# A mixer kernel in which the turns of the spatial gating weights are placed anew on TensorE

## The reference

```python
def _moe2_ref(x, w_in, g_ln, w_sg, b_sg, w_out) -> np.ndarray:
    h = x @ w_in
    c = np.float32(np.sqrt(2.0 / np.pi))
    h = 0.5 * h * (1.0 + np.tanh(c * (h + 0.044715 * h ** 3)))
    d_ff = h.shape[-1]
    u, v = (h[..., :d_ff // 2], h[..., d_ff // 2:])
    mu = np.mean(v, axis=-1, keepdims=True)
    var = np.mean((v - mu) ** 2, axis=-1, keepdims=True)
    v_n = (v - mu) / np.sqrt(var + 1e-06) * g_ln
    v_s = np.einsum('ts,bsd->btd', w_sg, v_n) + b_sg[None, :, None]
    gated = u * v_s
    return (x + gated @ w_out).astype(np.float32)
```

## Time and profile before

| | |
|---|---|
| time, median of 3 runs (lowest to highest) | 716.33 us (715.87 to 718.21) |
| the profiled execution's own time | 717.76 us |
| its span, first to last instruction | 715.9 us |
| PE busy | 706.1 us (99%) |
| DVE, ACT, POOL busy | 483.6, 382.8, 357.9 us |
| mean granted clock of TensorE | 0.998 of full speed |
| chain that ended last | PE 90%, DVE 7% |

### The profile page before, as it was taken

How to read it: one execution, slowest core, us unless ns; L and a number is a source line. 1 busy time by engine, 2 the same in 40 slices (tenths; PEclk the granted TensorE clock), 3 DMA queues, 4 the chain that set the end, 5 groups by cost and what they waited for, 6 DMA issues and landing times.

```text
span 715.9 us, 11889 instructions
## 1 busy us (share of the span) xinstructions
PE 706.1 (99%) x3933; PEld 596.4 (83%) x3933; DVE 483.6 (68%) x730; ACT 382.8 (53%) x719; POOL 357.9 (50%) x351
## 2 busy tenths in 40 slices
PE   8999999999999999999999999999999999999998
PEld 8766666666675899989899998998998899988997
DVE  8878787878875899986544567544434785648554
ACT  5778887788775436554444545444542563125311
POOL 4678778887887813134633262536633453016300
PEclk9999999999999999999999999999999999999999
DMA  5323232332333311032111112722104000110001
GB/s 117 69 61 84 64 72 62 76 68 60 73 74 114 112 53 59 1 109 67 60 60 60 59 60 84 250 79 60 30 2 168 1 1 1 44 45 1 1 30 60
DMA packets 70949, 45.60 MB, mean 64 GB/s; under 512 B 44740, under 2 KB 61304, under 8 KB 70392
## 3 DMA queue, kind: packets, MB, share of 16 engines
q1 hardware_dynamic: 69528, 41.38, 20.9%
q0 software_dynamic: 576, 3.43, 1.4%
q10 hardware_dynamic: 800, 0.20, 0.1%
HBM read 35.81 MB, written 3.15 MB: 54 GB/s over the span
## 4 chain that ended last, share of the span: by engine, by line
PE 90%; DVE 7%; ACT 1%; POOL 1%; issue 1%; SPq 0%; DMA 0%; POOLq 0%; ACTq 0%; DVEq 0%
PE PS L870 86%; DVE mneg L1870 1%; PE PS L899 1%; PE PS L1031 1%; PE PS L1339 1%; PE PS L1176 1%; PE PS L1348 1%; DVE yHL L1961 1%; DVE ops L1862 1%; DVE X L2069 1%; DVE un L2106 0%; DVE st L2094 0%; DVE vr L2246 0%; DVE X L2272 0%; DVE GL L2053 0%
## 5 line engine op out<-in xcount | busy, mean ns | idle before, releaser
L870 PE MATMUL PS<-ops 98*128 98x384 f32 (+1 forms) x576 | 133.8, 358 | 1.8 <-DVE mneg L1870 0.7
L870 PEld LDWEIGHTS PS<-ops 98*128 98x128 f32 (+1 forms) x576 | 95.8, 190 | 42.9 <-ACT E L1466 19.1
L1870 DVE TENSOR_REDUCE mneg<-PS 128x1 f32<-128x768 f32 x96 | 91.4, 956 | 38.3 <-PE PS L870 37.5
L1466 ACT ACTIVATE E<-PS 128x384 f32<-128x384 f32 x192 | 83.4, 486 | 45.8 <-PE PS L870 45.0
L698 POOL TENSOR_TENSOR esum<-esum,E 128x768 f32<-128x768 f32 x56 | 102.6, 1832 | 3.4 <-ACT E L1466 1.1
L683 POOL TENSOR_TENSOR W2L<-W2R,W2H 128x1024 fp32r<-128x1024 f32 x16 | 38.9, 2430 | 107.6 <-ACT W2H L1446 107.6
L2155 DVE SCALAR_TENSOR_TENSOR hL<-pre,hH 128x384 fp32r<-128x384 f32 x42 | 46.5, 1106 | 56.3 <-ACT hH L1709 56.3
L870 PE MATMUL PS<-BH,W1H 128*128 128x384 f32 x228 | 76.8, 337 | 0.3 <-DVE hL L2155 0.2
L870 PE MATMUL PS<-BH,W1L 128*128 128x384 f32 x228 | 76.9, 337 | 0.0
L870 PE MATMUL PS<-BL,W1H 128*128 128x384 f32 x228 | 76.1, 334 | 0.0
L870 PE MATMUL PS<-W2H,hH 128*128 128x512 f32 x192 | 75.4, 393 | 0.0
(11 more groups left out here) (230 smaller groups left out, 1625.8 us busy)
## 6 DMA issues: line engine op xcount, KB each, us to landing
W1R<-in_moe_w_ch_dram SPq DMA_DIRECT2D x32, 256.0 KB, 3.3
W2R<-in_moe_w_ch_dram SPq DMA_DIRECT2D x32, 256.0 KB, 2.9
ops<-ops SPq DMA_DIRECT2D x30, 192.0 KB, 2.9
qk<-in_k_dram SPq DMA_DIRECT2D x32, 96.0 KB, 2.5
vn<-in_v_dram SPq DMA_DIRECT2D x32, 96.0 KB, 2.5
out_dram<-X SPq DMA_DIRECT2D x12, 256.0 KB, 2.0
qk<-in_q_dram SPq DMA_DIRECT2D x30, 96.0 KB, 2.5
WsgR<-in_moe_w_sg_dram SPq DMA_DIRECT2D x1, 2304.0 KB, 8.3
```

The source lines that it names most:

```text
L870: return pe.matmul(dst, lhs, rhs, start=start, stop=stop, **kw)
L1466: act.activation(A["E"][:, e_slot(t, 0, kt), half(a)], PS[:, ST_BANK + a, 0:HALF], ACT.Exp, scale=EXP_SCALE).then_inc(exp_done, 1)
L1870: dve.tensor_reduce(A["mneg"][:, s, j:j + 1], PS[:, bank:bank + 2, 0:HALF], AX.XY, ALU.max, negate=True).then_inc(max_done, 1)
```

## The change

Two tables and the order of two calls are changed. In the first batch, t0 to t5 stood in five places behind the matmuls of V0, V1, V2, V3 and V4; they now stand in four places ahead of the matmuls of V1, V2, V3 and V4, right behind the turns of x. In the mixing, t6 to t11 stood in six places; they now stand in three, two blocks each.

```diff
         def turns_at(j):
-            return ((0,), (1,), (2,), (3,), (4, 5), ())[j]
+            return ((), (0,), (1,), (2, 3), (4, 5), ())[j]
 
         def turns_in_mix(stage, j):
-            return {(0, 0): (6,), (0, 1): (7,), (0, 2): (8,), (1, 0): (9,), (1, 1): (10,), (2, 0): (11,)}.get((stage, j), ())
+            return {(0, 0): (6, 7), (0, 3): (8, 9), (2, 0): (10, 11)}.get((stage, j), ())
...
                     if kind == V and j + 1 < T:
                         x_transposes(b, j + 1)
-                    hidden(b, i)
                     if b == 0 and kind == V:
                         for n in turns_at(j):
                             token_weights(n)
+                    hidden(b, i)
```

## The result

The changed kernel takes 717.84 us (median of 12 runs, 717.44 to 720.0) against 716.36 (12 runs of the kernel before beside it): the ratio is 1.0021, with a 95% interval of 1.0012 to 1.0031, so 0.9 to 2.2 us slower. Forecast was 717.6 and no change by the 0.3% bound; both hold. The profiled execution took 719.51 us, its span is 717.7.

A forecast was written before the change was run, and what follows sets the result against it. PE was taken as the bound, nearly throughout the chain from 548 to 606 us. The wait (+2.23), less transposes (0.71), a returned wait (0.16) and places (0.09), gave +1.27 on 716.33: 717.6 us, range 715.9 to 718.7.

The forecast's parts named there:

- The wait at t4 and t5: Ahead of V4, PE waits for DVE's lower parts of t2 and t3; V4 starts 2.23 us late, at 575.07.
- The six transposes behind V4: Behind V4 the six transposes of t4 and t5 are gone, -0.71 us, leaving PE 1.52 late from U3 on.
- The 0.16 is given back: At the mixing's start, PE's 0.16 us wait for a DVE GELU vanishes, as DVE falls back 1.05, PE 1.52.
- The mixing's places: In the mixing, three places fewer save 0.03 us each, 0.09 in all, within 0 to 0.57.
- The upper bound of 0.57: In the mixing, most that three places fewer could save, from 2.72 us left for six places, 0.45 each.
- The sum: Whole kernel: +2.23 - 0.71 - 0.16 - 0.09 = +1.27 us, giving 717.6 against the median of 716.33.
- t0 to t3 at cost 0: First-layer part: turning t0, t1 behind x2, x3 and t2, t3 behind x4 ahead of V3 costs 0.
- A: At the new wait ahead of t4, PE's clock falls: 1.75 us lost, kernel 3.0 slower, 719.3; chance 0.12.
- B: At t4 the wait is small or none because DVE reaches the lower parts earlier: 716.0 or 717.2; chance 0.13.
- C: Normalisation loop falls back further, holding PE at V5 or the mixing's start up to 1.5 us: 717.6 to 719.1; chance 0.06.
- D: A place costs far more than its transposes: six fewer, each over 0.6 us, would gain 2.1; chance 0.02.

The follow-up runs named there:

- mixing only: Kernel before with only the mixing's places t6 to t11 merged into three, t0 to t5 as before: 716.24 us, ratio 0.9995.
- t4 and t5 behind V4: Changed kernel with t4 and t5 put back behind V4's matmuls: 716.75 us, ratio 1.0004; with x4's lower part also moved early on DVE: 715.45 us, ratio 0.9986.
- x4's lower part early: Kernel before, places untouched, with DVE's lower part of x4 moved ahead of the centring of V2 in both batches: 715.31 us, ratio 0.9983.
- t2 sooner: Changed kernel with t2 ahead of V2, right behind t1, in place of V3: 721.05 us (4 runs), ratio 1.0058.

## Why the prediction was right, point by point

**The wait at t4 and t5** was forecast by its place, its releaser and its length (1.3 to 1.6 us of idle time; 1.55 measured), and V4 at 575.07; it came at 575.11. The two lower parts ended at 574.68 in place of 574.69 on the clock of before. Removing the wait removed the 1.63 us at U3, and shortening DVE's queue by 0.60 shortened it by 0.60, so the cause is shown.

**The six transposes behind V4** gave back 0.66 (2.29 less 1.63), where 0.71 was put down.

**"The 0.16 is given back" failed.** The step behind it was that DVE falls back by 1.05 and PE by 1.52, with no further wait of DVE on PE before the mixing. DVE's first row behind V4 did come 1.16 late (579.03 less 0.24, against 577.63), but DVE went on losing. Changed kernel, PE:

```profile
591.24 0.34 PE L870 MATMUL PS<-xTH,WinL 128*128 128x384 f32 x1
591.56 0.45 PE L870 MATMUL PS<-WsgH,VH 128*128 128x384 f32 x1
```

Again 0.32. No kernel here went below it. Where DVE hangs on PE again, the rows of ACT and DVE in the changed kernel show:

```profile
585.37 0.49 ACT L1768 ACTIVATE sq<-PS 128x384 f32<-128x384 f32 x1 [1.09 <-PE PS L870]
585.76 0.63 ACT L1773 ACTIVATE th<-sq 128x512 f32<-128x512 f32 x1
...
585.90 0.56 DVE L2277 SCALAR_TENSOR_TENSOR sq<-sq,PS 128x384 f32<-128x384 f32 x1
586.42 0.69 DVE L2285 SCALAR_TENSOR_TENSOR vr<-th,PS 128x512 f32<-128x512 f32 x1
...
589.10 0.55 DVE L2246 TENSOR_SCALAR vr<-vr,mv,rstd 128x512 f32<-128x512 f32 x1 [1.05 <-POOL rstd L857]
```

ACT's square of U4 starts when PE is done with U4, at 585.37. DVE's cubic step of U4 follows it, and V5's tanh stands behind it in ACT's queue. Then come V5's GELU and statistics, POOL's rstd, V5's centring, and in DVE's order two cubic steps and two GELUs, the last of which lets the mixing start at 591.56. That is 6.19 us from the square's start, and PE, with U5, U6 and U7 to do meanwhile, is ready 0.15 sooner. In seven more kernels here, all but the one before, "mixing only" and the two with t4 and t5 behind V4, it is the same: cubic step of U4 5.66 us and ACT's square 6.19 ahead of the mixing. In those four DVE does not stop at U4, and its own queue sets the time: 6.56 us from V5's cubic step to the mixing. That the kernel before was late by just this floor as well, 0.33 against 0.32, is chance, and it made the 0.16 look like a debt. Only what puts the loop later than the floor shows (0.47 and 0.19 of idle time above). This is read from the traces; no kernel here shortened the floor.

**The mixing's places**: 0.09 forecast, 0.09 to 0.13 measured. The upper bound of 0.57 was far off, and not only for the slow matmuls named there: the stretch of the earlier trace rows ends two matmuls behind the four stages, so it holds 74 matmuls and not 72, which leaves 2.38 us for six places, 0.40 each, and a bound of 0.24.

**The sum**: +2.23 - 0.71 - 0.16 - 0.09 = +1.27 was forecast, +2.29 - 0.66 + 0.01 - 0.09 = +1.55 measured behind the stages and +1.52 at the end. The mis-sized term is the 0.16, forecast to be given back and measured at nothing. Against the medians that is 717.84 for 717.6.

**t0 to t3 at cost 0** held in the changed kernel only, as the wait at t4 covers what they do. That t2's lower part leaves a free slot for a full one, 0.46 us on DVE's loop, I had worked into the wait and not seen as a cost of its own; with the wait removed it costs 0.48 us at the start of the mixing. The forecast came out without this term because the larger delay covered it.

**Rivals.** A: with 1.55 us of idle time the clock stayed at 1.00 in the profiled execution, and nine of the twelve executions have a mean clock of 1.000. With 2.61 us at the same kind of place it fell in the profiled execution and cost 1.5 us, and in two of the four executions it did not. So the mechanism is real, and one execution does not settle whether a wait brings it. B: no sign, DVE's rows stayed within 0.02 of where they were, since it is V1's and V2's ends, through POOL, that set them. C: the loop did fall back further than worked out, but without holding PE beyond the old 0.15. D: a place is worth 0.03 us. Its count of six places fewer was not the diff's: three are gone in the mixing and five in the first-layer part, where t0 to t5 now join the turns of x; the sum does not use it.

## What to carry to other kernels

A ring of two buffers that is filled ahead of a stage needs its frees from two stages back, not from the one just ended. Here moving a fill one stage earlier in a queue turned an empty wait into 1.55 us, though no work was added. Gathering small batches on the bounding engine is worth only the measured cost of a switch (0.03 us here), so look first where it makes the in-order engine stand. When a wait is due to another engine's queue, look for idle time ahead in that queue and put independent work there; that was worth 0.9 to 1.7 us by the trace, where the change itself cost 1.5. And when a wait seems to be the debt of an engine that runs late, ask where that engine next waits for the first one: behind that point the debt is not carried on.

## What the runs showed of the hardware

The same idle time lets TensorE's clock fall in one execution and not in another. All twelve kernels are the same up to the third block, and in the profiled executions of four (before, changed, mixing only, t4 and t5 behind V4) the clock fell near 31 us, in those of the other eight not. Of the kernel before, 27.6 to 31.0 us holds 2.29 us of PE work, and the 3.5 us behind it ran at 0.51 of the clock. In the run with x4's lower part early, whose program is the same there:

```profile
27.60:31.00 3.40, 2.28 (x14) 1.00 0.00 0
31.00:34.50 3.50, 3.50 (x20) 1.00 0.18 40
```

PE did 20 matmuls in place of 11, and everything behind is 1.5 us earlier from 37 us on (1.77 at 552.8 us, of which 0.26 were there at 30 us). A mean clock of 1.000 or of 0.998 or less over the span tells whether an execution holds such a fall, though not where: in the run with t2 sooner the mean of 0.997 is from the fall at 561 us, and its stretch behind 31 us ran at 1.00. So profiles of a kernel are to be compared by sections, or that difference is read as an effect of the edit.

Turns of 128 x 128 in float32 cost 0.11 to 0.12 us each from start to start, in three, in four or in six, between matmuls in the rounded float32 format: a change from the one kind to the other costs at most 0.03 us a place. Behind a wait they cost more: t4 with t5 took 0.84 us from t4's start to V4's (574.51 to 575.35), where the same six took 0.61 behind V4 in the kernel before.
